# Five broadcast copies and three small additions moved from VectorE to GpSimd in a linear-attention and soft-MoE kernel

## What is computed

```python
def _attn_ref(q, k, v, g_norm):                      # 8 batches, 8 heads, 576 tokens, 64 wide
    kv = np.einsum('bhsd,bhse->bhde', k, v)
    out = np.einsum('bhsd,bhde->bhse', q, kv)
    rms = np.sqrt(np.mean(out * out, axis=-1, keepdims=True) + 1e-06)
    return out / rms * g_norm

def _moe_ref(x, phi, w1, w2):                        # x: 4608 x 512, 8 experts of 4 slots, F = 1024
    logits = x @ phi                                 # 4608 x 32
    d = np.exp(logits - logits.max(0, keepdims=True))
    d /= d.sum(0, keepdims=True) + 1e-09
    slot_input = (d.T @ x).reshape(E, S_per_e, D)
    for e in range(E):
        slot_out[e] = np.maximum(slot_input[e] @ w1[e], 0.0) @ w2[e]
    c = np.exp(logits - logits.max(1, keepdims=True))
    c /= c.sum(1, keepdims=True) + 1e-09
    return c @ slot_out.reshape(n_slots, D)
```

## Time and profile before

| | before |
|---|---|
| median of 3 runs | 172.13 us (171.98 to 172.15) |
| profiled execution | 172.24 us |
| its span | 170.8 us |
| mean granted clock of TensorE | 0.975 of full |
| PE busy | 148.4 us (87%) |
| DVE busy | 85.7 us (50%), 184 instructions |
| ACT busy | 89.0 us (52%), 232 instructions |
| POOL busy | 60.6 us (36%), 76 instructions |
| DMA | 71.65 MB, mean 419 GB/s |
| chain that ended last, by engine | PE 43%, DMA 31%, ACT 10%, DVE 6% of the span |

### The profile page before, as it was taken

How to read it: one execution, slowest core, us unless ns; L and a number is a source line. 1 busy time by engine, 2 the same in 40 slices (tenths; PEclk the granted TensorE clock), 3 DMA queues, 4 the chain that set the end, 5 groups by cost and what they waited for, 6 DMA issues and landing times.

```text
span 170.8 us, 4205 instructions
## 1 busy us (share of the span) xinstructions
PE 148.4 (87%) x1821; PEld 103.4 (61%) x1821; DVE 85.7 (50%) x184; ACT 89.0 (52%) x232; POOL 60.6 (36%) x76
## 2 busy tenths in 40 slices
PE   7978998979999999999899998899989799988100
PEld 3547887969767878797697673366557443445000
DVE  1111437743669166762946698636885046229100
ACT  3114778795887686859749866213221044328100
POOL 7000246757177735477382678700000004000000
PEclk9999999999999999999999999999999999999955
DMA  5999999999999999999899999999999989999995
GB/s 183 436 450 407 482 411 419 430 502 414 414 405 468 414 444 479 418 429 418 384 420 465 460 426 395 470 412 387 418 430 445 455 387 414 429 413 430 423 452 236
DMA packets 3357, 71.65 MB, mean 419 GB/s; under 512 B 678, under 2 KB 678, under 8 KB 810
## 3 DMA queue, kind: packets, MB, share of 16 engines
q1 hardware_dynamic: 2986, 71.18, 97.4%
q0 software_dynamic: 352, 0.20, 0.4%
HBM read 61.94 MB, written 9.44 MB: 418 GB/s over the span
## 4 chain that ended last, share of the span: by engine, by line
PE 43%; DMA 31%; ACT 10%; DVE 6%; SPq 1%; issue 1%
PE psum L205 43%; DMA arena<-in_kv_dram 20%; DMA arena<-in_w_dram 11%; ACT bd L205 3%; ACT sq L205 2%; ACT arena L205 2%; DVE ms L205 2%; DVE logits L205 1%; SPq L205 1%; ACT part L205 1%; ACT d L205 1%; DVE part L205 1%; ACT r L205 1%; DVE acc L205 0%; DVE r L205 0%
## 5 line engine op out<-in xcount | busy, mean ns | idle before, releaser
L205 PE MATMUL psum<-bd,arena 128*128 128x192 f32 (+1 forms) x320 | 56.8, 336 | 2.2 <-ACT arena L205 1.0
L205 PEld LDWEIGHTS psum<-bd,arena 128*128 128x128 f32 (+1 forms) x320 | 45.5, 179 | 10.5 <-ACT arena L205 3.5
L205 PE MATMUL psum<-arena 128*64 128x64 f32 (+2 forms) x896 | 36.0, 270 | 2.9 <-DMA arena<-in_kv_dram 1.8
L205 DVE TENSOR_REDUCE ms<-sq 128x16 f32<-128x1024 f32 (+1 forms) x19 | 22.0, 1162 | 29.9 <-ACT sq L205 29.7
L205 PEld LDWEIGHTS psum<-arena 128*64 128x64 f32 (+2 forms) x896 | 27.5, 129 | 13.8 <-issue 4.1
L205 POOL TENSOR_TENSOR part<-part,r 128x512 f32<-128x512 f32 x17 | 17.8, 1047 | 49.7 <-DVE r L205 49.7
L205 POOL TENSOR_TENSOR arena<-arena,r 128x512 f32<-128x512 f32 x34 | 34.7, 1042 | 0.0
L205 ACT COPY arena<-psum 128x512 f32<-128x512 f32 (+2 forms) x48 | 30.8, 651 | 7.1 <-PE psum L205 7.1
L205 ACT ACTIVATE sq<-psum 128x512 f32<-128x512 f32 x36 | 21.5, 596 | 9.5 <-PE psum L205 9.3
L205 ACT COPY part<-psum 128x256 f32<-128x256 f32 (+1 forms) x38 | 13.7, 360 | 10.5 <-DVE part L205 9.3
L205 DVE TENSOR_REDUCE logits<-part 128x64 f32<-128x512 f32 (+1 forms) x17 | 17.2, 1013 | 0.0
(11 more groups left out here) (75 smaller groups left out, 103.4 us busy)
## 6 DMA issues: line engine op xcount, KB each, us to landing
arena<-in_kv_dram SPq DMA_DIRECT2D x1, 6912.0 KB, 30.4
arena<-in_t_dram SPq DMA_DIRECT2D x1, 6912.0 KB, 25.2
arena<-in_w_dram SPq DMA_DIRECT2D x1, 6912.0 KB, 28.0
arena<-in_w_dram SPq DMA_DIRECT2D x1, 6144.0 KB, 24.2
arena<-in_w_dram SPq DMA_DIRECT2D x3, 2048.0 KB, 18.8
arena<-in_w_dram SPq DMA_DIRECT2D x1, 5120.0 KB, 18.6
arena<-in_w_dram SPq DMA_DIRECT2D x1, 4352.0 KB, 31.8
arena<-in_w_dram SPq DMA_DIRECT2D x1, 4096.0 KB, 23.3
```

Source lines behind the costliest of these rows:

```text
L205: inst = getattr(engine, method)(*args, **kwargs)
```

## The change

`group_max` makes its fourfold copy on GpSimd instead of VectorE (five instructions in a run, for groups 0 to 4), and `combine` makes its addition of the constant there (three instructions). Places in the program, operands and sizes are the same; the waits that follow from the new engine are put in by the recorder.

```diff
@@ -595,7 +595,7 @@
         )
         if n is None:
             tops[G] = wk.tile([P, 4, NS], F32, tag="top", name=f"top{G}", bufs=1)
-            nc.vector.tensor_copy(out=tops[G], in_=L[:, at + GROUPS[G]].unsqueeze(1).to_broadcast([P, 4, NS]))
+            nc.gpsimd.tensor_copy(out=tops[G], in_=L[:, at + GROUPS[G]].unsqueeze(1).to_broadcast([P, 4, NS]))
 
     def last_max(G):
         at = pos(g0[G])
@@ -843,7 +843,7 @@
         nc.scalar.activation(C, C, AF.Exp)
         cs = wk.tile([P, W], F32, tag="cs", name=f"cs{k}")
         nc.vector.tensor_reduce(out=cs, in_=C, axis=AX.X, op=ALU.add)
-        nc.vector.tensor_scalar_add(cs, cs, EPS_SUM)
+        nc.gpsimd.tensor_scalar_add(cs, cs, EPS_SUM)
         nc.vector.reciprocal(cs, cs)
         c = wk.tile([P, W, NS], F32, tag="part", name=f"c{k}", bufs=3)
         nc.vector.tensor_tensor(out=c, in0=C, in1=cs.unsqueeze(2).to_broadcast([P, W, NS]), op=ALU.mult)
```

## The result

The changed kernel takes 172.25 us (median of 22 runs, 171.88 to 172.58), the kernel before, timed beside it, 171.81 us (22 runs, 171.58 to 172.22): a ratio of 1.0020, 95% interval 1.0012 to 1.0028. So the change makes the kernel slower by 0.2%, some 0.35 us by the ratio (the two medians lie 0.44 us apart). The figure 172.25 lies inside the forecast range, but the forecast of no change did not hold.

The account below looks back on a forecast made before the run. DMA was taken as the bound; PE's delay of 0.9 + 0.4 = 1.3 us stayed under 3.1 us of slack, so 172.24 + 0 gave a forecast of 172.1 us, range 171.8 to 172.7 us.

Parts of the forecast that it names:

- The bound by DMA: Whole kernel: packets of SP's queue fill 97.4% of the time of 16 DMA engines, so DMA sets the span.
- The slack at the last store: At the end: the last store, issued at 159.27 us, could come 1.6 us later without moving the end.
- PE's two waits for weights: Before 124.81 and 134.56 us: waits of 0.62 and 0.91 us, said to swallow up to 1.53 us of PE's delay.
- a slower result through PE's delay: Rival: handoffs make PE's delay exceed 3.1 us and the last store late, 173.1 us; chance 0.13, including a milder form.
- Maximum to PE: At each changed copy: time from group maximum to PE's load, 0.31 us before, 0.29 us later in all after.
- the handoff to PE: Behind each copy: time from POOL's end to PE's start, taken as 0.10 us from the POOL to DVE handoff.
- a wait behind a step for r: At each copy: POOL waits for DVE's first step for r, starting at about 0.20 us instead of 0.08 us.
- PE's waits for the top tile: At the group copies: 2.2 us in all before, expected to grow by 0.5 to 2 us.
- POOL's addition: In the three combines: 128x13 addition on POOL taken as 0.18 us, between 0.10 and 0.25 us.
- The three waits of DVE: In the combines: DVE waits for cs on POOL three times, some 0.3 us each.
- the 1.4 us around it: Outside the span: the profiled execution's 172.24 us taken as 170.8 us of span plus 1.4 us.
- the rivals: Handoffs over the slack, slower, 0.13; DVE is the bound, faster, 170.9 us, 0.09; DVE not relieved, inside the forecast's 0.78.

Follow-up runs that it names:

- e11: Kernel before with newton's three steps replaced by one copy of the root, 36 VectorE instructions fewer (148); ratio to before 1.0007.
- e13: Kernel before without the refinement of the root, plus 28 one-column fills at the start of VectorE's stream (176 instructions); ratio to before 1.0027.
- e16: Kernel before without the refinement of the root, plus 12 one-column fills at the start of VectorE's stream (160 instructions); ratio to before 0.9999.
- e12: Kernel before with twelve filler matmuls on PE ahead of the last gather; ratio to before 1.0011.
- e7: The change plus eight one-column fills on VectorE where the eight moved instructions were (184 instructions); ratio to before 1.0001.
- e3: The whole change timed again, copies and additions both on GpSimd, against the kernel before; 172.20 us, ratio 1.0021.
- e8: Kernel before with the five copies and three additions removed from VectorE, none added on GpSimd, PE 35 matmuls more; ratio to before 1.0016.
- e10: The change plus eight one-column fills at the start of VectorE's stream (184 instructions); ratio to before 0.9998.
- e9: The change plus three one-column fills on VectorE, in the combines only (179 instructions); ratio to before 1.0010.
- e2: Kernel before with only the three additions moved to GpSimd, copies still on VectorE (181 instructions); 171.79 us, ratio 1.0001.

## Why the prediction was wrong

**What held.** The bound by DMA held: e11 and e13 to e16 leave most of `newton` out, e12 adds some 2 us of delay near the end, and no span moves by more than 0.3 us. The slack at the last store was put at 1.6 us from two issues and two landings; it measured 1.6 to 1.9 us. Whatever part of PE's 0.3 us before the experts is the change's was taken up, but not quite as the text said: of PE's two waits for weights the first shrank by 0.23 us (0.62 to 0.39 us), and the second did not (0.91 to 0.97 us), because its load was issued later too and spent less time in the queue. The chance of a slower result through PE's delay was rightly small: e7 has all eight handoffs and issues these weights at 115.89 us, and costs nothing.

**Sizes.** POOL's copy took 0.29 us (0.30 predicted). Maximum to PE grew by 0.10 us, where I had 0.29 us: the handoff to PE was 0.06 us and not 0.10 us, and the 0.12 us that I had charged for a wait behind a step for r did not come. I had put that step from 0.03 to 0.20 us behind the maximum. It began 0.08 us before the maximum's recorded end and was over 0.09 us behind it, about when POOL could start in any case, so these rows do not show whether POOL would wait for a step. PE's waits for the top tile therefore grew by 0.3 us, less than the 0.5 us named as the least. In the other direction DVE did wait. The first of the pair behind POOL's copy, in the trace after from 83.41 to 83.5 us:

```profile
83.42 0.27 DVE L205 SCALAR_TENSOR_TENSOR r<-r 128x16 f32<-128x16 f32 x1
```

It took 0.27 us, where such a step takes 0.18 us on average in the kernel before, and it ended at 83.69 us, 0.04 us behind POOL's copy (83.65 us), just as the step of 0.55 us ends 0.04 us behind POOL's scalings. The same 0.27 us stand behind the copies at 51.28 and 98.48 us. The Trainium skill, SBUF — State Buffer, section "SBUF: two separate sides", states an exclusive lock: whichever of a GpSimd operation that reads SBUF and a VectorE operation with two SBUF inputs starts first keeps the other out for its whole instruction. With GpSimd first these traces agree with it, for a copy of 0.29 us (price 0.09 us for the pair) as for a long scaling; with VectorE first no row here shows it. POOL's addition took 0.25 us (0.18 predicted, 0.25 the upper end). The three waits of DVE were 1.1 us in all, as named in advance (some 0.3 us each).

**The step that failed** is "The profiled execution took 172.24 us (span 170.8 us and 1.4 us around it), and 172.24 + 0". Every term of the sum was about the span; the 1.4 us around it I carried over as a constant. They are not: they are 1.33 us or 1.7 us, depending on how long VectorE's program is, and the change shortened it from 184 to 176 instructions, into the band that costs. That is the whole cost: 0.36 us outside the span (e3), 0.02 us inside, with an error of 0.05 us. Of the rivals none named it. That 172.25 us lies so near the forecast of 172.1 us is luck in part: the forecast stood on three runs with a median of 172.13 us, and over 22 runs the kernel before has 171.81 us. The closest thing in the prediction is its last sentence, that an effect with all issues in place is one for which none of the steps allows. The packets on q14 stood on the page of before, five of them, and I did not ask for whom the last one came.

**What stays open.** That the cost goes with VectorE's length, whatever the instructions, is shown (e7, e8, e10, e13). That a late instruction fetch is the mechanism is an inference: the packet behind the span is seen in one trace (e9), and in the four with 176 instructions none is seen. Nor does the packet simply come when VectorE reaches some instruction: in the kernel before VectorE has started 168 of its 184 instructions when it comes, in e2 all 181, which is not the same place, counted from the start or from the end. Why 172 and fewer cost nothing is open too; their traces show no fifth packet, just as those with 176. Why the two kernels with 179 differ (1.44 and 1.57 us) is not known, nor whether the programs of ACT, PE and POOL have such bands (POOL: not at 84 and 108). No version beat the kernel before: with DMA full, less work on VectorE has nothing to give. The change together with fills up to the old length (e7, e10) equals it.

## What to carry to other kernels

Where DMA is full and each issue stands well ahead of its queue, as here, neither moving small instructions between engines nor a microsecond of delay changed the span; read the slack from an issue and the landing ahead of it before any cost is added up. Keep the device time and the span apart in each run, for an edit that only changes how many instructions an engine has cost a third of a microsecond outside the span here. Where a difference of 0.2% has no place in the trace, compare time minus span first, and try a few empty instructions on the engine whose program changed, before a story is made of it.

## What was not expected of the hardware

Time minus span has two levels here, 1.33 and 1.69 us, sharp to some 0.1 us from run to run. It goes with the number of VectorE's instructions and is not monotonic: 184, 181, 172, 168, 160 and 148 give the low level, 176 the high one (three different kernels), and 179 values between. In one trace (e9) a packet of instructions comes 1.3 us behind the last instruction of the span. And a short VectorE step with two SBUF inputs that starts under POOL's copy of 0.29 us ends 0.04 us behind that copy: 0.27 us instead of 0.18 us.
